# Attention scores as one fp32 matmul of 64 rows per head, and ten weight chunks split beside attention

## What is computed

```python
# attention: B=2, H=8 heads, S=768, D=64, n_global=8, n_local=96
scores = q @ k.T / sqrt(D)
keep   = is_global | is_local        # first 8 keys, or 0 <= query - key < 96
scores = where(keep, scores - slope[h] * dist, -1e9)
x      = softmax(scores) @ v         # [B, S, 512] once the heads are side by side
# block 1: token mixing, then channel mixing
u = x + (relu(x.T @ w_tok1) @ w_tok2).T
x = u + relu(u @ w_ch1) @ w_ch2
# block 2
theta = x @ w_theta
u   = x + w_tok_r @ (x * cos(theta)) + w_tok_i @ (x * sin(theta))
out = u + relu(u @ w_ch)
```

## Time and profile before

| | |
|---|---|
| time, median of 3 runs | 559.53 us (559.32 to 559.75) |
| span of the profiled execution | 558.8 us |
| PE busy | 520.8 us, 93% |
| DVE busy | 296.1 us, 53% |
| ACT busy | 184.5 us, 33% |
| POOL busy | 149.8 us, 27% |

### The profile page before, as it was taken

The page is one execution under the profiler, slowest core; times in us unless marked ns, Lnnn a source line. Parts: engine busy times, 40 slices in busy tenths (PEclk is TensorE's granted clock), DMA queues, the critical chain, the costliest instruction groups (busy, mean ns, idle before and its releaser), DMA issues.

```text
span 558.8 us, 8294 instructions
## 1 busy us (share of the span) xinstructions
PE 520.8 (93%) x3060; PEld 480.2 (86%) x3060; DVE 296.1 (53%) x709; ACT 184.5 (33%) x474; POOL 149.8 (27%) x143
## 2 busy tenths in 40 slices
PE   2979978976999999999999999999879999999997
PEld 2869868954899999997999999998768899888887
DVE  5999999866511132116511133418874483756442
ACT  3879888931211112112211113332142231233120
POOL 6656665569600000000400002242800040000040
PEclk9999998986999999999999999999979999999999
DMA  6636564413400000000200001123100002000002
GB/s 249 251 106 247 193 208 140 149 60 114 132 1 1 0 1 1 0 1 0 75 40 0 1 0 57 23 91 96 38 1 0 1 18 82 15 1 1 2 16 97
DMA packets 9262, 35.08 MB, mean 63 GB/s; under 512 B 1152, under 2 KB 3200, under 8 KB 7808
## 3 DMA queue, kind: packets, MB, share of 16 engines
q1 hardware_dynamic: 9216, 34.48, 18.3%
HBM read 31.33 MB, written 3.15 MB: 62 GB/s over the span
## 4 chain that ended last, share of the span: by engine, by line
PE 78%; DVE 14%; issue 5%; ACT 2%; POOL 1%; DMA 1%; DVEq 0%; ACTq 0%
PE bank L261 67%; PE bank L1112 4%; PE bank L1077 2%; DVE wsplit L777 2%; DVE tile L891 2%; DVE scores L850 2%; PE bank L1093 1%; DVE third L891 1%; PE bank L1185 1%; PE bank L1212 1%; DVE gprobs L795 1%; PE bank L1140 1%; DVE wsplit L788 1%; ACT wsplit L668 1%; DVE zb L928 1%
## 5 line engine op out<-in xcount | busy, mean ns | idle before, releaser
L261 PE MATMUL bank<-split,wsplit 128*128 128x384 f32 x768 | 144.0, 339 | 0.8 <-DVE act_raw L1026 0.8
L261 PEld LDWEIGHTS bank<-split,wsplit 128*128 128x128 f32 x768 | 135.2, 188 | 1.0 <-DVE act_raw L1026 1.0
L261 PE MATMUL bank<-hid,wsplit 128*128 128x384 f32 (+1 forms) x648 | 128.3, 346 | 0.0
L261 PEld LDWEIGHTS bank<-hid,wsplit 128*128 128x128 f32 x648 | 115.3, 189 | 3.7 <-DVE hid L959 0.6
L261 PE MATMUL bank<-wsplit,zs 128*128 128x512 f32 (+1 forms) x576 | 105.3, 343 | 0.2 <-DVE zs L941 0.2
L986 DVE SCALAR_TENSOR_TENSOR hid<-bank,hid 128x384 fp32r<-128x384 f32 x48 | 26.8, 557 | 142.9 <-ACT hid L707 142.9
L261 PEld LDWEIGHTS bank<-wsplit,zs 128*128 128x128 f32 x576 | 90.5, 191 | 13.7 <-issue 0.4
L560 POOL TENSOR_TENSOR wsplit<-wraw,wsplit 128x1536 fp32r<-128x1536 f32 (+1 forms) x16 | 52.5, 3279 | 99.5 <-ACT wsplit L668 98.7
L707 ACT ACTIVATE hid<-bank 128x384 fp32r<-128x384 f32 x48 | 23.6, 491 | 151.8 <-PE bank L261 151.8
L629 ACT ACTIVATE probs<-scores,nmax 128x232 f32<-128x232 f32 (+1 forms) x96 | 44.8, 467 | 17.9 <-DVE nmax L850 17.0
L1112 PEld LDWEIGHTS bank<-vt,probsT 128*128 128x128 f32 (+1 forms) x352 | 41.7, 187 | 9.2 <-ACT probsT L582 7.8
(11 more groups left out here) (101 smaller groups left out, 538.5 us busy)
## 6 DMA issues: line engine op xcount, KB each, us to landing
wraw<-weights SPq DMA_DIRECT2D x16, 768.0 KB, 4.2
qk_raw<-qk SPq DMA_DIRECT2D x11, 1056.0 KB, 4.9
vt<-v SPq DMA_DIRECT2D x12, 256.0 KB, 2.6
out<-act_raw SPq DMA_DIRECT2D x16, 192.0 KB, 1.9
wraw<-weights SPq DMA_DIRECT2D x4, 512.0 KB, 3.5
qk_raw<-qk SPq DMA_DIRECT2D x1, 792.0 KB, 5.3
vg<-v_first SPq DMA_DIRECT2D x2, 256.0 KB, 5.3
qk_raw<-qk SPq DMA_DIRECT2D x1, 264.0 KB, 3.4
```

What stands on the lines that cost most here:

```text
L261: mm = pe.matmul(dst, lhs(a), rhs(c), start=first and i == 0, stop=last and i == 2, skip_group_check=True)
```

## The change

1. `head_scores` has one plain fp32 matmul for each head, over 64 rows. The two heads of a pair lie in the two row halves of the same columns (`q_in[rows, ...]`, `k_in[rows, ...]`, rows 0 to 63 and 64 to 127), as the DMA brings them. `queries_hi`, `keys_hi`, `keys_lo`, `split_first` and the POOL subtraction L533 are gone, with their semaphores.
2. The queries have three buffers (`QBUFS`) and are loaded two units ahead; each key tile of a batch has its own place, so nothing is written twice. Queries and keys are not loaded in double any more, and are two DMAs a unit in place of one. The counts are loaded third instead of first.
3. No weight slot is borrowed; `vg_split` has a buffer of its own. All ten chunks of block 1 are loaded and split during attention, one a unit in units 0 to 9, and POOL splits a chunk as one copy and one subtraction of 1536 columns.

```diff
-BESIDE = [0, 1, 4, 7]
-SLICES = 3
+BESIDE = SLOTS
...
             def load_queries_keys(n):
                 b, t = divmod(n, T)
-                first = 2 if n == 0 else 0
-                if n >= 2:
-                    sp.wait_ge(q_lo, PAIRS * (n - 1))
-                    sp.wait_ge(k_lo, splits(n - 2))
-                sp.dma_start(qk_raw[:, n % 2, first:], qk[b, t, :, first:]).then_inc(qk_in[n % 2], 16)
-
+                first = 1 if n == 0 else 0
+                if n >= QBUFS:
+                    sp.wait_ge(s_ready, 2 * PAIRS * (n - QBUFS + 1))
+                sp.dma_start(q_in[:, n % QBUFS, first:], qk[b, t, :, first:, 0:P]).then_inc(
+                    q_landed[n % QBUFS], 16)
+                sp.dma_start(k_in[:, first:, t * KW:(t + 1) * KW], qk[b, t, :, first:, P:]).then_inc(
+                    k_landed[n % QBUFS], 16)
+
+            sp.dma_start(q_in[:, 0, 0], qk[0, 0, :, 0, 0:P]).then_inc(pair_in, 16)
+            sp.dma_start(k_in[:, 0, 0:KW], qk[0, 0, :, 0, P:]).then_inc(pair_in, 16)
             sp.dma_start(counts[:, :], both_counts.partition_broadcast(P)).then_inc(counts_in, 16)
-            sp.dma_start(qk_raw[:, 0, 0:2], qk[0, 0, :, 0:2]).then_inc(pair_in, 16)
-            load_queries_keys(0)
+            for n in range(QBUFS - 1):
+                load_queries_keys(n)
...
-                if n in BESIDE:
-                    load_weight(BESIDE.index(n))
+                if n + QBUFS - 1 < UNITS:
+                    load_queries_keys(n + QBUFS - 1)
+                if n < BESIDE:
+                    load_weight(n)
...
+            def split_weight(i):
+                slot, width = ORDER[i] % SLOTS, WIDTHS[ORDER[i]]
+                raw = wraw[:, i % 2, 0:width]
+                pool.wait_ge(w_in[i % 2], 16 * (i // 2 + 1))
+                link(pool.tensor_copy(w_at(slot, 0, 0, width), raw))
+                pool.tensor_tensor(w_at(slot, 1, 0, width), raw, w_at(slot, 0, 0, width).bitcast(F32),
+                                   ALU.subtract).then_inc(w_ready, 1)
+
+            for i in range(BESIDE):
+                split_weight(i)
...
-                    h = 2 * p + e
-                    for i in range(2):
-                        mm = pe.matmul(S_BANK[m % 2][e][:, first:WIN], q_split[:, n % 2, h, :],
-                                       k_split[:, i, h, keys], start=i == 0, stop=i == 1)
-                    mm.then_inc(s_ready, 1)
+                    rows = slice(e * D, (e + 1) * D)
+                    pe.matmul(S_BANK[m % 2][e][:, first:WIN], q_in[rows, n % QBUFS, p, :],
+                              k_in[rows, p, keys], start=True, stop=True).then_inc(s_ready, 1)
```

More of the change, by code:

```diff
@@ L50 @@
 SLOPES = [2.0 ** (-8.0 * (h + 1) / H) for h in range(H)]
[L52 to L53 removed]
+QBUFS = 3
 CHUNK = 1536
@@ L263, in three @@
             return mm
-        def places(t):
-            return [PLACES[t]] if t != RING - 1 else [RING - 1, 0]
-        def splits(n, p=PAIRS - 1):
-            return PAIRS * sum(len(places(i % T)) for i in range(n)) + (p + 1) * len(places(n % T))
         UNITS = B * T
@@ L612, in _ @@
                 act.activation(bias[:, h, :], c_base, ACT.Copy, scale=SLOPES[h]).then_inc(bias_ready, 1)
-            for p in range(1, PAIRS):
-                keys_hi(0, p)
             for m in range(STEPS + 3):
@@ L1064, in head_scores @@
                 n, p = divmod(m, PAIRS)
-                place = PLACES[n % T]
-                if n % T == 0:
-                    first, keys = P, slice(place * KW, (place + 1) * KW)
-                else:
-                    first, keys = UNSEEN, slice((place - 1) * KW + G + UNSEEN, (place + 1) * KW)
-                pe.wait_ge(k_lo, splits(n, p))
-                pe.wait_ge(q_lo, m + 1)
+                t = n % T
+                if t == 0:
+                    first, keys = P, slice(0, KW)
+                else:
+                    first, keys = UNSEEN, slice((t - 1) * KW + G + UNSEEN, (t + 1) * KW)
+                if m == 0:
+                    pe.wait_ge(pair_in, 32)
+                else:
+                    pe.wait_ge(q_landed[n % QBUFS], 16 * (n // QBUFS + 1))
+                    pe.wait_ge(k_landed[n % QBUFS], 16 * (n // QBUFS + 1))
                 if m >= 2:
```

119 lines of the change are left out of this document (17 added, 102 removed).

## The result

The changed kernel takes **571.16 us** (median of 4 runs, 567.52 to 579.88). Before, measured beside it on the same chip, it is 559.64 (559.32 to 561.32). The ratio is 1.0175, with an interval from 1.0116 to 1.0233: slower, where 554.3 was forecast. The changed kernel's runs lie 12 us apart and those of before 2 us. The profiled execution is the longest of the four, 579.88 us, with a span of 578.1.

What follows compares the result with a forecast made beforehand. Attention was taken as near the limit of both DVE and PE, with POOL limiting the stretch behind it. Terms: -2.6 + 8 - 1 - 9.0 - 0.6 = -5.2; 558.8 - 5.2 + 0.7 = 554.3 us, range 543 to 564.

Steps and rivals of the forecast that it cites:

- the PE term: PE in attention: fp32 scores add 1.12 us a unit, yet PE-bound units make 83.4 us where 86 stood, -2.6 us.
- a granted clock under 1 through attention: PE's clock in attention: listed among the signs that would show the forecast wrong, with no size or chance given.
- Scores at full clock: PE's scores in attention: four records at two cycles a column, 0.78 us a step for 0.50 before.
- the rival with overlap: PE's scores: one head's second record beside the next's first, 539 with POOL's waits absorbed (0.20 for 538 to 549), otherwise 552.
- Draining at the switch of rows: PE in attention: switching between 64 and 128 rows drains it, 15 us in 44 steps, 564 us; chance 0.15.
- The lock's price: DVE in attention: `gather` waits for the end of POOL's long subtraction, 0.7 to 0.8 us a chunk reaching PE, +8 us.
- The start: First units: counts some 0.8 us later, step 4's scores 1.5 to 2 earlier, partly given back at 1.2 GHz; -1 us.
- Behind attention: From attention's end to token mixing: POOL has only tile 0 left, 12.3 us instead of 21.3, -9.0 us.
- The clock's part: Token mixing's 18 first products: with PE running on, 4.2 us instead of 5.01 less its tail, -0.6 us.
- DVE, ACT and the loads: Attention: about 38 us leave DVE and L593 leaves ACT, worth nothing alone; loads two units ahead stay hidden.

Runs made afterwards that it cites:

- 128 rows: The changed kernel with each score matmul over all 128 rows instead of 64, summing both heads of a pair, whole chunks kept: 554.56 us, ratio 0.9898.
- the second run of the changed kernel: The changed kernel measured once more with no edit: 576.82 us (567.93 to 590.99, 4 runs) beside 560.01 for before; its profile has a span of 569.1.
- the slices: The changed kernel, 64-row scores kept, with each chunk split by three copies and three subtractions of 512 columns: 546.29 us, ratio 0.9774.
- its two variants: The kernel before with only its scores changed to one fp32 matmul per head, over 64 rows (574.89 us) or 128 rows (565.73 us).
- the single wait on purpose: The kernel with slices and 64-row scores, plus one added PE wait in step 20 for a copy needed only later: 560.02 us against 546.29.

## Why the prediction was wrong

**The failed step is the PE term: "nine full units at 7.33 + 1.12 = 8.45", with "PE is then the limit throughout".** It took 2.4 GHz for granted from unit 2 on, because PE would be busy. PE was busy, and in the profiled run the clock stayed at 1.2 GHz for units 1 to 3 and 7 to 9, so that units of 14.45 to 14.67 us stand where 8.45 was forecast. With 128 rows in the same kernel this doesn't happen. This was named as something that would show the forecast wrong ("a granted clock under 1 through attention") but had neither a rival nor a price.

Point by point:

- *Scores at full clock.* The forecast had 0.78 us a step for one record after the other. In the second run of the changed kernel the chain at full clock has:

```profile
67.07 0.59 PE bank L994 x4
67.66 0.54 PE bank L1009 x4
68.20 0.73 PE bank L1028 x8
```

  The forecast was of four records at 0.193; the rival with overlap had three times 0.193, which is 0.58. The time is the rival's, but not its order: by the starts of the records, in this trace and in that of the slices, the first records of the two heads start 7 ns apart, and so do the second ones, 0.29 to 0.30 us later. So the heads run side by side throughout, and a pair takes 0.3 us where a single record over 128 rows takes 0.2. By the Trainium skill, TensorE: Matmul & The Clock Gate, Part 3 (The mechanism), matmuls in different row groups run concurrently; the trace agrees, 0.59 us here against 0.84 from the scores' start to the transposes' with 128 rows. The transposes behind take 0.54 on the chain where they took 0.39 and 0.39 with 128 rows, 0.15 more. So a unit is 8.05 us, not 8.45. At 1.2 GHz it is 14.5.
- *Draining at the switch of rows.* It was priced at 0.34 us a step, and decided from 0.12. Those 0.15 us are the place where it could be. By the starts of the records they lie at both edges: from the last record of the values to the first score it is 0.18 us with 64 rows and 0.09 with 128, and from the first transpose to the second 0.14 and 0.09. The time from scores to the end of the transposes is 1.13 us with 64 rows and 1.23 with 128, so the overlap outweighs it. Whether the 0.15 are a drain wasn't tried.
- *The lock's price.* Priced at 8 us, 0.8 a chunk, by way of `gather`. With 128 rows it is 13.8 us in the medians, of which 10.2 lie in the ten units, 1.0 for a chunk, and 2.5 behind the start of token mixing, where the same edit slices the later chunks. The mechanism was right: `gather` and L732 end with POOL's subtraction. The size was a little low. In the second run of the changed kernel L732 (three times) and the bias copy L765 (once) are held for over 3 us too, which the forecast left out; whether that is the 0.2 a chunk wasn't tried. What the step lacked is that such a wait can also bring down the clock, which with 64 rows can cost more than the wait itself. The Trainium skill, SBUF — State Buffer, section Who interferes with whom, names `copy`, `cast` and `tensor_scalar` among those that can contend with GpSimd for the whole of an instruction; the 3.16 us of a `tensor_scalar` of 128x8 agree.
- *Where the clock holds, the sum comes out.* With 128 rows and whole chunks, units 2 to 10 take 83.2 us, 9.24 each; the prediction had 8.45 + 0.8 = 9.25 for a full unit. That kernel takes 554.6 us, and 554.3 was forecast. The agreement is closer than the terms deserve (units 6 and 7 are shorter than the others, and the lock costs more), but the prediction describes the change with 128-row scores, not the one made.
- *The start.* The counts come at 4.29 instead of 3.55, 0.7 later (forecast 0.8), and step 4's scores at 15.1 instead of 17.41, 2.3 earlier (forecast 1.5 to 2). Then unit 1 takes 12.11 us at 1.2 GHz, and unit 2 begins at 27.19, 1.2 us later than before instead of 1 earlier. With 128 rows it begins at 23.27. The sign failed for the same reason as the PE term.
- *Behind attention.* -8.7 for -9.0. `tile_to_lo` takes 0.69 us where it took 3.48. It was argued from rows of before, and it holds in every run of the changed kernel and its variants. The clock's part, -0.6, was 0.9.
- *DVE, ACT and the loads* were worth nothing and cost nothing, as forecast. A chunk lands in 6.0 us instead of 4.2, which no wait shows after the start.

## What to carry to other kernels

Filling only half of TensorE's rows saves loads and splits, and may even stream faster, but the clock must be checked along with it: with 64-row matmuls a wait of 1.5 us was followed by up to 51 us at half the clock, and the low level of the start lasted 26 to 96 us instead of 15 to 17. Either keep PE free of such waits, or pad the operand with zeros to 128 rows. Work moved beside a stage is cheap only if its longest instruction is short: cutting POOL's subtractions from 3.44 to 1.29 us was worth 14 us with a steady clock and 25 to 31 with an unsteady one (medians, with about 2.5 us of it behind attention). And a sum built on a clock of the old kernel needs the question what in the change could alter it.

## What the runs showed of the hardware

- The low level of the start. With 64-row scores the first record of full clock comes at 26.0, 26.5, 27.0, 56.0, 58.4 and 96.5 us in six profiles, and at 216.7, behind attention, where both heads use rows 0 to 63. With scores over 128 rows it comes at 14.6, 14.6, 15.8, 16.0 and 17.1. In the kernel before it comes at 23.6. PE is busy almost throughout from 12 us on in all but the kernel before and its two variants, which have waits of 0.4 to 0.8 us until 20.
- Falls inside attention. With 64-row scores the clock fell behind every wait of PE of 0.91 us or more at full clock, eight in five profiles (0.91 to 1.92 us), and the low level lasted 3.4, 3.4, 6.8, 6.8, 13.7, 24, 44 and 51 us, with PE busy nearly throughout. With fp32 scores over 128 rows it fell behind 1.99 us, for 3.4 us, and not behind 1.23, 1.23 and 1.03. In the kernel before it fell behind 1.57 us, for 3.4 us, and not behind 1.38 and 1.05. So long stretches are seen with 64 rows alone, but short ones too, and falls with 128 rows are few.
- What of the scores' use of the array the clock follows is open. The two heads side by side, fp32 as such, the new staging and zeros among the data are ruled out by runs here. Not separated are the number of rows and the change between 64-row and 128-row matmuls, twice a step: every 64-row kernel here has both. What ends a slow stretch, and why some are short, these runs don't tell either.
- Whether the clock stays low differs from run to run: with the single wait on purpose one run of ten has a clock of 0.997 and takes 543.4 us.
- At the lower level, 1.2 GHz, a score group of 0.66 us takes 1.15 and a unit of 8.05 takes 14.5: 1.7 and 1.8 times as long, with PE busy throughout in both.
- An fp32 product of 232 columns leaves two records. Over 128 rows at 2.4 GHz they start 196 ns apart; on one row half at 1.2 GHz they start 387 ns apart. Two cycles for each column are 193 and 387 ns, as with the transposes.
